# Attention with tiles of two heads on the array's row halves, and outputs in two blocks a pair

## The reference

```python
scores = scale * np.matmul(q, k.transpose(0, 1, 3, 2))       # 4 x 8 x 576 x 576
x = (log1p(abs(i - j)) / log1p(max(i, 1)))[..., None]
bias = np.maximum(x @ w1 + b1, 0.0) @ w2                     # per head
scores = scores + bias.transpose(2, 0, 1)[None]
attn = np.exp(scores - max);  attn = attn / (sum(attn) + 1e-09)
out = np.matmul(attn, v)                                     # heads side by side: 2304 x 512
h = np.maximum(np.maximum(x @ w1, x @ w2), x @ w3) @ w_out   # 512 -> 768 -> 512
g = h2 = h @ w_in;  g = 0 below -1, h2 above 1, (h2 + 1)**2 / 4 between
result = g @ w_out2                                          # 512 -> 2048 -> 512
```

## Time and profile before

| | us |
|---|---|
| median of 3 runs (1085.83 to 1088.53) | 1086.34 |
| the profiled execution | 1088.05 |
| its span, first to last instruction | 1086.1 |
| outside the span | 1.95 |
| TensorE busy in the span | 1045.2 (96%) |
| VectorE busy | 551.9 (51%) |
| ScalarE busy | 504.3 (46%) |
| GpSimd busy | 307.6 (28%) |
| bias stage | 0 to 62 |
| attention | 62 to 381 |
| the two layers | 381 to 1086 |

### The profile page before, as it was taken

The page is one execution under the profiler, slowest core; times in us unless marked ns, Lnnn a source line. Parts: engine busy times, 40 slices in busy tenths (PEclk is TensorE's granted clock), DMA queues, the critical chain, the costliest instruction groups (busy, mean ns, idle before and its releaser), DMA issues.

```text
span 1086.1 us, 18925 instructions
## 1 busy us (share of the span) xinstructions
PE 1045.2 (96%) x6936; PEld 925.6 (85%) x6936; DVE 551.9 (51%) x1314; ACT 504.3 (46%) x1081; POOL 307.6 (28%) x536
## 2 busy tenths in 40 slices
PE   6789999999999999999999999999999999999998
PEld 3467777777777699999999999989998989989897
DVE  8867777767777523222312232775444444444543
ACT  7887676666766533121212122554344343443433
POOL 5037776767767463000000033650000000000000
PEclk9989999999999999999999999999999999999999
DMA  5871332422431132000000012310000000000000
GB/s 132 244 214 37 95 94 56 133 52 58 132 76 42 51 116 79 1 0 0 0 0 0 0 46 72 98 59 30 1 1 29 0 29 0 0 29 0 30 1 30
DMA packets 93157, 56.00 MB, mean 52 GB/s; under 512 B 61345, under 2 KB 78753, under 8 KB 93089
## 3 DMA queue, kind: packets, MB, share of 16 engines
q1 hardware_dynamic: 92992, 55.11, 17.8%
q10 hardware_dynamic: 96, 0.00, 0.0%
HBM read 39.46 MB, written 15.63 MB: 51 GB/s over the span
## 4 chain that ended last, share of the span: by engine, by line
PE 86%; DVE 9%; issue 2%; ACT 1%; DMA 1%; POOL 0%; SPq 0%; ACTq 0%
PE ps L1012 39%; PE ps L1072 18%; PE ps L1040 7%; PE ps L918 7%; PE ps L938 5%; PE ps L950 5%; DVE xT L802 3%; DVE s_sb L751 3%; PE ps L903 2%; DVE k_lo L769 2%; PE ps L998 2%; DVE pt_t L760 1%; PE ps L977 1%; DMA bias_h<-bias_scratch 0%; DVE p_t L740 0%
## 5 line engine op out<-in xcount | busy, mean ns | idle before, releaser
L1012 PE MATMUL ps<-x_hi,w_all 128*128 128x384 f32 x1632 | 437.1, 335 | 0.3 <-issue 0.3
L1012 PEld LDWEIGHTS ps<-x_hi,w_all 128*128 128x128 f32 x1632 | 296.9, 188 | 5.3 <-issue 1.0
L1012 PE MATMUL ps<-x_lo,w_all 128*128 128x384 f32 x816 | 273.2, 335 | 0.0
L1072 PE MATMUL ps<-w_all,g_hi 128*128 128x512 f32 x576 | 179.7, 393 | 0.0
L751 DVE CUSTOM_DVE_ANT_0 s_sb<-ps,bias_h 128x576 f32<-128x576 f32 (+1 forms) x160 | 120.2, 752 | 78.4 <-PE ps L938 60.8
L504 POOL TENSOR_TENSOR w_all<-raw,w_all 128x256 fp32r<-128x256 f32 x104 | 80.4, 806 | 274.4 <-ACT w_all L627 270.1
L1012 PEld LDWEIGHTS ps<-x_lo,w_all 128*128 128x128 f32 x816 | 153.2, 188 | 3.9
L583 ACT ACTIVATE probs<-s_sb,row_min 128x576 f32<-128x576 f32 (+1 forms) x160 | 124.6, 779 | 34.4 <-DVE row_min L751 32.9
L471 POOL TENSOR_SCALAR probs<-probs,row_inv 128x512 f32<-128x512 f32 (+1 forms) x160 | 108.2, 690 | 106.2 <-DVE row_inv L731 106.2
L1072 PEld LDWEIGHTS ps<-w_all,g_hi 128*128 128x128 f32 x576 | 106.3, 188 | 19.2 <-issue 1.2
L1072 PE MATMUL ps<-w_all,g_lo 128*128 128x512 f32 x288 | 113.9, 395 | 0.0
(11 more groups left out here) (87 smaller groups left out, 1391.0 us busy)
## 6 DMA issues: line engine op xcount, KB each, us to landing
bias_scratch<-p_t SPq DMA_DIRECT2D x36, 296.0 KB, 3.7
bias_h<-bias_scratch SPq DMA_DIRECT2D x32, 288.0 KB, 4.2
raw<-in_moe_w_out SPq DMA_DIRECT2D x22, 256.0 KB, 3.0
raw<-in_moe_w SPq DMA_DIRECT2D x18, 256.0 KB, 3.2
out<-o_sb SPq DMA_DIRECT2D x18, 256.0 KB, 2.1
q_in<-in_q SPq DMA_DIRECT2D x32, 128.0 KB, 2.4
k_in<-in_k SPq DMA_DIRECT2D x32, 128.0 KB, 2.4
v_in<-in_v SPq DMA_DIRECT2D x32, 128.0 KB, 2.3
```

What stands on the lines that cost most here:

```text
L1012: last = pe.matmul(ps[:, bank, 0:BLK], w[:, at:at + P], x[:, kt, :], start=(kt == 0 and n == 0), stop=(kt == KT - 1 and n == 2))
L1072: last = pe.matmul(ps[:, O_BANK + t, :], g[:, ft % 4, t * P:(t + 1) * P], w[:, wout_d(ft):wout_d(ft) + DM], start=(opens and i == 0), stop ...
```

## The change

Each tile now holds the same 128 rows of **both heads of a pair**. A slot (`slot(w)`, 80 of them and three more at the end) works on one such tile; GROUPS = 16 pairs have five slots each. In what follows:

- **Loads.** `q_in` and `k_in` hold the two heads side by side, 64 columns each, so that one transpose turns both: head 0 lands on partitions 0 to 63, head 1 on 64 to 127 (`turn_in`). The high and low parts are formed after the turn, from `tqk`, by GpSimd (`high_turned`, `low_turned`); the copies `q_dup` and `k_dup` are gone. k of head 1 is loaded with its last 64 rows first, so its columns are rotated, and its bias too (two loads).
- **Scores.** A head's contraction has 64 rows now, on its half of the array's rows. Three passes (high by high, high by low, low by high), two column halves, two heads: 12 matmuls a tile, heads in turn, into four banks (0 and 1, 2 and 3). VectorE adds the bias of both heads; TensorE's next scores wait for both.
- **Probabilities.** `probs` holds both heads side by side, 1152 columns. GpSimd normalises 576 columns a head. Three slots later (`LAG`) the middle 128 columns (tail of head 0, rotated tail of head 1) are turned by one transpose into bank 7, together with one tile of q and of k for a later pair; the other 8 blocks of 128 columns are turned by 64 rows at a time, upper row half into bank 4, lower into bank 5, 16 transposes. ScalarE copies bank 4 and 7, VectorE bank 5.
- **Outputs.** The two halves of a pair's output, the same 10 instructions each as before (20 matmuls in the trace), come in the slots of tile 1 and tile 3 of the next pair, into bank 6; VectorE copies them.
- Denominators move from VectorE to GpSimd. The bias is stored with another scale.
- At the end x_lo and the low weights stand behind VectorE's last slot.

TensorE, steady attention, before: the last two tiles of an even step and the first tile of the next; `k_hi,q_s` are scores, `ident,probs` the transposed probabilities, `p_t,v_in` and `pt_t,v_in` the outputs.

```diff
+    GROUPS = PAIRS // 2
+    NU = GROUPS * NT
+    LAG = 3
+    RING = LAG + 2
...
+        X_BANK, Y_BANK_P, O_BANK_A, T_BANK = 4, 5, 6, 7
...
+        def turns_of(w):
+
+            at = (0, 2, 4, 5)[w] if w < 4 else w + 2
+            return [j for j in range(NT + at, NT + at + (2 if w < 2 else 1)) if j < NU]
...
+            def high_turned(w):
+
+                for n, j in enumerate(turns_of(w)):
+                    i, t = j // NT, j % NT
+                    par, at = staged(w, n)
+                    pool.wait_ge(t_cp, w + 1)
+                    if i >= 2:
+                        pool.wait_ge(s_ps, 2 * NT * (i - 1))
...
+            def slot(w):
+
+                high_turned(w)
+                if w < 2:
+                    low_turned(w)
+                if w:
+                    normalise(w - 1)
+                if w < NU:
+                    denominators(w)
+                if w >= 2:
+                    low_turned(w)
...
+            def slot(w):
+                copy_turned(w)
+                if w < NU:
+                    exponent(w, 0)
+                if tile_of(w) is not None:
+                    copy_upper(tile_of(w))
+                if w < NU:
+                    exponent(w, 1)
...
+            def slot(w):
+                i, t = w // NT, w % NT
+                if t == 2 and i >= 1:
+                    output(i - 1, 0)
+                if t == 4 and i >= 1:
+                    output(i - 1, 1)
+                if w < NU:
+                    add_bias(w, 0)
+                    add_bias(w, 1)
+                    if w:
+                        inverse(w - 1)
+                if w == NU:
+                    inverse(NU - 1)
+                if tile_of(w) is not None and tile_of(w) % NT < T:
+                    copy_lower(tile_of(w))
...
-            for m in STEPS[1:]:
-                step(m)
-                if m == PAIRS:
-                    split_x(0, c_x_hi, c_x_ok)
-                    low_weights(0)
-            dve.wait_ge(o_ok, PAIRS)
+            for w in SLOTS:
+                slot(w)
+            split_x(0, c_x_hi, c_x_ok)
+            low_weights(0)
+            output(GROUPS - 1, 1)
             low_weights(2)
...
+            def scores(u):
+                i, t = u // NT, u % NT
+                if t == 0:
+                    pe.wait_ge(lo_ok, NT * (i + 1))
+                if u == T:
+                    pe.wait_ge(pads_zero, 2)
+                if u:
+                    pe.wait_ge(s_bias, 2 * u)
+                for c in range(2):
+                    for n, (a, b) in enumerate(((qk_hi, qk_hi), (qk_hi, qk_lo), (qk_lo, qk_hi))):
+                        ends = [pe.matmul(ps[:, 2 * h + c, 0:HC], a[HALVES[h], i % 2, 0, t * P:(t + 1) * P],
+                                          b[HALVES[h], i % 2, 1, c * HC:(c + 1) * HC], start=(n == 0), stop=(n == 2))
+                                for h in range(2)]
+                for end in ends:
+                    end.then_inc(s_ps, 1)
+
+            def turn_probs(u):
+                t, r = u % NT, u % RING
+                pe.wait_ge(p_norm, 2 * u + 2)
+                pe.wait_ge(p_cx, u)
+                pe.wait_ge(p_cy, y_count(u))
+                for c in range(2 * T):
+                    at = c % T * P + c // T * (S + HALF)
+                    ends = [pe.transpose(ps[:, X_BANK + e, c * HALF:(c + 1) * HALF], probs[HALVES[e], r, at:at + P],
+                                         ident[HALVES[e], HALVES[e]]) for e in range(row_halves(t))]
+                ends[0].then_inc(px_ps, 1)
+                if t < T:
+                    ends[1].then_inc(py_ps, 1)
...
+            VALUES = {1: (0, range(NT)), 3: (1, range(NT))}
...
+            def slot(w):
+                i, t = w // NT, w % NT
+                if w < NU:
+                    scores(w)
+                if w == 0:
+                    pe.wait_ge(bias_sb, NSUP)
+                turn_rest(w)
+                if tile_of(w) is not None:
+                    turn_probs(tile_of(w))
+                if i >= 1 and t in VALUES:
+                    values(i - 1, *VALUES[t])
...
-            for m in STEPS[1:]:
-                step(m)
-                if m == PAIRS:
-                    first_item(0)
+            for w in SLOTS:
+                slot(w)
+            first_item(0)
+            values(GROUPS - 1, 1, range(NT))
             first_item(1)
```

More of the change, by code:

```diff
@@ L506, in low_weights @@
                 last.then_inc(w_ok, 1)
[L508 to L511 removed]
+            for w in range(NU + 1):
+                slot(w)
             pool.wait_ge(w_ok, 1)
@@ new lines, in exponent @@
+            def exponent(u, h):
+                n, r = rows[u % NT], u % RING
+                act.wait_ge(s_bias, 2 * u + h + 1)
+                if u >= RING and h == 0:
+                    act.wait_ge(px_ps, u - RING + 1)
+                    act.wait_ge(py_ps, y_count(u - RING + 1))
+                    act.wait_ge(t_ps, u - RING + LAG + 1)
+                act.activation(probs[0:n, r, h * S:(h + 1) * S], s_sb[0:n, (2 * u + h) % 4, :], ACT.Exp, scale=-1.0,
+                               bias=row_min[0:n, r, h:h + 1], accum_out=row_sum[0:n, r, h:h + 1]).then_inc(p_exp, 1)
@@ new lines, in turn_rest @@
+            def turn_rest(w):
+                u, js = tile_of(w), turns_of(w)
+                if w:
+                    pe.wait_ge(t_cp, w)
+                if u is not None:
+                    n = rows[u % NT]
+                    pe.wait_ge(p_norm, 2 * u + 2)
+                    last = pe.transpose(ps[:, T_BANK, 0:n], probs[0:n, u % RING, MAIN:MAIN + P], ident[0:n, 0:n])
+                for n, j in enumerate(js):
+                    if j % NT == 0:
+                        pe.wait_ge(qk_in[j // NT % 2], 144 * (j // NT // 2 + 1))
+                    at = 2 * n * P if w < 2 else P
+                    turn_in(T_BANK, at, q_in, j // NT % 2, j % NT)
+                    last = turn_in(T_BANK, at + P, k_in, j // NT % 2, j % NT)
+                last.then_inc(t_ps, 1)
@@ L914, in outputs @@
                     if 2 * i + half >= 1:
                         pe.wait_ge(o_ok, 2 * i + half)
-                    for kt in range(NT):
-                        for h in range(2):
-                            last = pe.matmul(ps[h * HALF:(h + 1) * HALF, O_BANK_A, 0:cols.stop - cols.start],
-                                             v_in[:, i % 2, h, kt, :],
-                                             pt_t[:, i % 2, cols] if kt == T else p_t[:, i % 2, h, kt, cols],
-                                             start=(kt == 0), stop=(kt == T))
@@ L974, in step @@
-                if par == 0 and has(m, 2):
-                    bank = open_slot("tail")
-                    for t in range(T):
-                        last = pe.transpose(ps[:, bank, t * P:(t + 1) * P],
-                                            p_tail[:, t, :, :].rearrange("p a d -> p (a d)"), ident[:, :])
-                    last.then_inc(t_ps, 1)
+                for kt in units:
+                    for h in range(2):
+                        last = pe.matmul(ps[h * HALF:(h + 1) * HALF, O_BANK_A, 0:cols.stop - cols.start],
+                                         v_in[:, i % 2, h, kt, :],
+                                         tqk[:, i % 2, 0, cols] if kt == T else p_t[:, i % 2, h, kt, cols],
+                                         start=(kt == 0), stop=(kt == T))
```

563 lines of the change are left out of this document (234 added, 329 removed).

## The result

| us | before | after | forecast |
|---|---|---|---|
| median | 1086.57 (4 runs) | 1075.22 (1074.67 to 1077.05, 4 runs) | 1061 (1044 to 1085) |
| ratio to before, 95% interval | | 0.9896 [0.9878, 0.9913] | 0.976 |
| profiled execution, its span | 1088.05, 1086.1 | 1075.25, 1073.1 | 1062.6 |
| first scores start | 62.44 | 60.69 | 62.4 |
| second product of the next layer starts | 381.09 | 367.97 | 355.6 |

It is faster, by 11.4 us and not by 25.5. The second product stands 13.1 us earlier in the trace, 12.4 less than the forecast had it; behind it nothing changed. So the missing time is in the attention and around it.

What follows compares the result with a forecast made beforehand. TensorE bounds steady attention at 19.38 us a pair; 15 new pairs at 17.6 us, plus start and end, bring the second product to 355.6 against 381.1, 25.5 us less: 1061 us, range 1044 to 1085.

Steps and rivals of the forecast that it cites:

- Score pair: TensorE, attention scores: two matmuls on two row halves side by side take 0.135 us, bounds 0.135 and 0.27.
- slots without an output: Steady attention: a loop of scores, tail, VectorE's two additions and the way back to TensorE, 2.6 us a slot.
- the blocking wait: GpSimd, slot of tile 3: high part waits for tile 4's scores, holding up normalisation and denominators; 0.3 us a pair.
- no overlap: Rival, TensorE: row halves do not overlap at all, a pair 22.4 us with the stall, 1137 us; chance 0.08.
- transposes one after the other: Rival, TensorE: transpose halves not side by side, 0.96 instead of 0.56 us, 12 us in all, 1073; chance 0.14.
- loads that bind: Rival, TensorE: weight loads follow each other, score pair 0.19 us, slot 0.33 longer, 1087 us; chance 0.05.
- the 19 us more: Scores: at the skill's 3.07 of 4, a pair takes 0.176 us instead of 0.135, kernel some 19 us slower.
- SyncE "at nothing, give or take 1 us": Bias stage: nine loads instead of four ahead of the first store cost nothing, give or take 1 us.
- Pair 0 was put at 14.6: Attention's first pair, without outputs: 5 x 2.6 = 13 us, and 1.6 for a stretch at half clock.
- the end at 14.6: Attention's end: tile 78 3.2, output half 2.4, VectorE's next-layer parts 3.8, product 2.3, last half 2.9 us.
- TensorE waiting 3 us for low weights: Sign at the attention's end: TensorE waits 3 us for low weights before the first product.
- rival "clock": Short slots: TensorE's idle 0.5 of 2.6 us lowers its clock to 1.2 GHz, 27 us lost, 1088; chance 0.07.

Runs made afterwards that it cites:

- the one-half runs: Changed kernel with both heads' score matmuls on row half 0: 1161.34 us; changed kernel with both transposes of a pair on row half 0: 1099.68 us.
- the low parts spread: Kernel with all three repairs, but low weights behind slot 73, x_lo halved behind 76 and 78, ScalarE's high weights behind 71: 1055.44 us.
- six apart: Changed kernel with all six score matmuls of head 0, then all six of head 1: 1117.82 us, ratio 1.0255.
- The three repairs: Changed kernel with loads by GpSimd, its high part behind normalisation and denominators, next-layer preparation moved into last slots, two products before last output: 1057.29 us.
- Three apart: Changed kernel with three score passes of head 0, then three of head 1, in each column half: 1076.06 us, ratio 0.9901.

## Why the prediction was wrong, and where it was right

**The direction and the steady stage were right.** Score pair 0.135 forecast, 0.133 measured; transposes pair 0.07 and 0.08 over a whole group (0.063 inside it); slots without an output 2.6 and 2.63 to 2.90 (2.63 to 2.68 once the blocking wait was gone), bounded as worked out by scores, additions and the way back; slots with an output 4.5 and 5.0 against 4.6 and 4.95; a pair 17.6 against 17.77. The blocking wait was 0.46 where it said 0.3. The rivals of no overlap, of transposes one after the other, and of loads that bind are refuted by the starts in the timeline, and the one-half runs price the first two: 86 and 24 us over the changed kernel, where the rivals had 76 and 12 over the forecast. In the steady slots at a full grant these rivals' sizes hold (0.76 a slot, 0.95 a pair); they left the clock out. The Trainium skill, "TensorE: Matmul & The Clock Gate", section "Measured speedup vs the span model", made a score pair an estimated 0.176 us; two halves gave the full factor of two here, so the 19 us more that it implied are not there.

**The first step that failed: SyncE "at nothing, give or take 1 us".** It counted the loads of the bias stage and asked whether they delay stores. It did not follow the queue to its last nine loads, and to when they are needed: the first transposes of the third pair come in slot 3, 9 us after the first scores. Pair 0 was put at 14.6 and took 21.8. Taking the loads out of the queue brought it to 15.8, and 6 us back.

**The second: the end at 14.6 (17.2 from the last scores).** Its terms were each sized at full clock and from a row where they lay in steady work. Measured, the way to the first output half took 1.2 us more (1.1 of it ScalarE's x_hi ahead of a copy), and the output half 1.6, the product 1.9 and the last half 0.9 more at half clock; VectorE's part came out about as forecast, 3.6 for 3.8. Of 5.4 us, 4.4 are clock. The forecast had the gap that the second fall came in ("TensorE waiting 3 us for low weights") and put no clock against it; the first fall came behind the waits for the turning of tile 78, which are inside its 3.2. Where the work behind the second gap was moved ahead, product and last output took 2.3 and 2.8 again.

**What the rival "clock" had right and wrong.** It placed the danger in the short slots. In the steady ones, where TensorE idles 0.5 to 0.9 of 2.6 us, the grant stayed 1.00 throughout. In pair 0 it did fall in the short slots, at 65.8 us, behind waits of 1.0 and 1.1 us and ahead of the wait of 5.62; the forecast had 1.6 us for that. At the end it fell behind waits of 1.80 and 1.69 us and within one of 2.9, and with the low parts spread, where the longest was 1.2, it did not fall. It also fell in the steady part of two kernels with more matmul time in a slot (0.93 and 0.92), mostly in the slot of tile 3. The wait ahead of that slot was 0.86 us with both heads on one half, as in the changed kernel (0.89), and 1.24 with six apart. Why the first of these fell is open; no run here tells it apart.

Together: +7.2 and +5.4 for the two failed steps; +1.5 for the steady part, where the larger blocking wait costs 2.3 over 14 pairs and the last pair, which turns no q and k, is 0.8 shorter; and -1.7 for the start, which is no more than one execution differs from the next by (60.4 to 62.3). The three repairs gave 17.9 us, more than the 12.4 missing, because they also remove two things that the forecast had accepted: 0.3 us of blocking wait in each pair (4.5 us) and a part of the wait for low weights.

## What to carry to other kernels

Follow each queue to its last entry before the pipeline is full, and set the time of its issue against the first use; a load "a pair ahead" in steady work is not ahead in the first. At both ends of a stage price each wait twice: its length, and what the half clock behind it costs (here 1.6 us behind the first and 2.8 behind the second), and fill it with whatever matmuls are ready. When a timeline names one releaser, look which other one ends next behind it before you move it: that one bounds the gain.

## What the runs showed of the hardware

- Two matmuls on two row halves of 64 start mostly 2 to 4 ns apart and cost one (0.133 us for 288 columns); on one row half, 0.265. For transposes of 64 columns it is 0.063 and 0.125 us the pair inside a group, 0.71 and 1.18 us busy for the whole group of 16.
- The halves need not alternate in the program, and a matmul can start ahead of earlier ones of the other half. Three apart they still pair up, 10 ns apart; six apart, the second half's first starts 0.37 us late, with the first half's third.
- GpSimd issued its loads at 0.54 to 0.98 us each (18, nine in 6.1 and nine in 6.5 us), SyncE at 0.52 to 0.63, and the pair's first scores did not suffer from it (61.07 against 60.69).
